# Expert stage on Trainium2: x2's sums in steps, rounding next to its ReLU, two products of h in the second product's banks, three banks for it, first copies by ScalarE

## What is computed

```python
def _moe2_ref(x, w_gate, w1, w2):          # x 3072x384, w1 8x384x1024, w2 8x1024x384
    logits = x @ w_gate
    logits = logits - logits.max()
    P = np.exp(logits)
    for _ in range(8):
        P /= P.sum(1, keepdims=True) + 1e-09
        P /= P.sum(0, keepdims=True) + 1e-09
        P *= N / E
    out = np.zeros((N, D), dtype=np.float32)
    for e in range(E):
        h = np.maximum(x @ w1[e], 0.0)
        ye = h @ w2[e]
        out += P[:, e:e + 1] * ye
    return out
```

## Time and profile before

| | us |
|---|---|
| runs of the kernel before | 2412.17, 2411.98, 2409.96 |
| median | 2411.98 |
| the profiled execution: time / span | 2413.01 / 2411.2 |
| TensorE matmuls busy in the span | 2256.0 |
| VectorE / ScalarE / GpSimd busy | 1743.3 / 979.0 / 503.9 |
| mean granted TensorE clock, share of full | 0.985 |

### The profile page before, as it was taken

The page is one execution under the profiler, slowest core; times in us unless marked ns, Lnnn a source line. Parts: engine busy times, 40 slices in busy tenths (PEclk is TensorE's granted clock), DMA queues, the critical chain, the costliest instruction groups (busy, mean ns, idle before and its releaser), DMA issues.

```text
span 2411.2 us, 38296 instructions
## 1 busy us (share of the span) xinstructions
PE 2256.0 (94%) x13723; PEld 2084.9 (86%) x13723; DVE 1743.3 (72%) x3098; ACT 979.0 (41%) x1669; POOL 503.9 (21%) x325
## 2 busy tenths in 40 slices
PE   2699999999998989999998999999998999999999
PEld 2689999999998878888887888888887888888888
DVE  6888888888864676666776676666667666766665
ACT  3455555555554333333333333333333333333332
POOL 0000000000000222232331233223232223332232
PEclk9799999999999999999999999999999999999999
DMA  3211111111112221111111121111101210111111
GB/s 105 82 42 51 49 48 48 48 47 48 47 35 93 65 80 53 53 52 39 40 52 53 53 105 53 53 52 52 50 28 52 79 51 29 53 52 53 52 53 27
DMA packets 70727, 131.35 MB, mean 54 GB/s; under 512 B 5512, under 2 KB 36488, under 8 KB 70536
## 3 DMA queue, kind: packets, MB, share of 16 engines
q1 hardware_dynamic: 70536, 129.14, 16.2%
HBM read 114.96 MB, written 14.16 MB: 54 GB/s over the span
## 4 chain that ended last, share of the span: by engine, by line
issue 41%; PE 29%; DVE 11%; POOL 11%; ACT 8%; POOLq 0%; DMA 0%; DVEq 0%; ACTq 0%; SPq 0%
POOL h_l L553 6%; PE bank L1402 5%; POOL w_l L548 5%; PE bank L1404 5%; PE bank L1403 5%; PE bank L1562 2%; PE bank L1564 2%; PE bank L1563 2%; PE bank L1383 2%; PE bank L1389 2%; PE bank L1388 2%; PE bank L1393 1%; ACT ubuf L637 1%; ACT ubuf L639 1%; ACT ubuf L635 1%
## 5 line engine op out<-in xcount | busy, mean ns | idle before, releaser
L1562 PE MATMUL bank<-w_h,h_h 128*128 128x384 f32 x1536 | 526.8, 343 | 38.5 <-DVE acc L1221 22.3
L1564 PE MATMUL bank<-w_h,h_l 128*128 128x384 f32 x1536 | 517.8, 337 | 0.0
L1563 PE MATMUL bank<-w_l,h_h 128*128 128x384 f32 x1536 | 517.5, 337 | 0.0
L553 POOL TENSOR_TENSOR h_l<-u_s,h_h 128x512 fp32r<-128x512 f32 x192 | 244.6, 1295 | 1046.9 <-ACT h_h L768 1046.9
L1402 PE MATMUL bank<-x_h,w_h 128*128 128x512 f32 x1056 | 414.7, 393 | 3.4 <-DVE h_l L1200 3.4
L1403 PE MATMUL bank<-x_l,w_h 128*128 128x512 f32 x1056 | 414.3, 392 | 0.0
L1404 PE MATMUL bank<-x_h,w_l 128*128 128x512 f32 x1056 | 413.2, 391 | 0.0
L1221 DVE SCALAR_TENSOR_TENSOR acc<-bank,prob,acc 128x384 f32<-128x384 f32 x352 | 215.9, 614 | 252.5 <-PE bank L1564 252.5
L1562 PEld LDWEIGHTS bank<-w_h,h_h 128*128 128x128 f32 x1536 | 291.1, 189 | 63.3 <-POOL h_l L553 29.3
L757 ACT ACTIVATE p_s<-bank 128x512 f32<-128x512 f32 x96 | 57.5, 599 | 603.9 <-PE bank L1404 603.9
L1563 PEld LDWEIGHTS bank<-w_l,h_h 128*128 128x128 f32 x1536 | 291.2, 190 | 2.0
(11 more groups left out here) (163 smaller groups left out, 4118.0 us busy)
## 6 DMA issues: line engine op xcount, KB each, us to landing
stage<-w_ SPq DMA_DIRECT2D x48, 768.0 KB, 6.5
w_raw<-w_ SPq DMA_DIRECT2D x96, 384.0 KB, 3.5
qb<-q_in_ SPq DMA_DIRECT2D x24, 192.0 KB
kb<-k_in_ SPq DMA_DIRECT2D x24, 192.0 KB
vb<-v_in_ SPq DMA_DIRECT2D x24, 192.0 KB
x_hi<-x2h_s SPq DMA_DIRECT2D x36, 128.0 KB, 1.8
x_lo<-x2l_s SPq DMA_DIRECT2D x36, 128.0 KB, 1.8
x_h<-x_hi SPq DMA_DIRECT2D x3, 1536.0 KB, 11.0
```

Source lines behind the costliest of these rows:

```text
L553: pool.tensor_tensor(tiles_of(h_l, name), group_sum(name), tiles_of(h_h, name).bitcast(F32), ALU.subtract).then_inc(hl_done, 1)
L1562: pe.matmul(dst, h_h[:, f, t_], w2h[:, fw], start=n == 0, stop=False)
L1563: pe.matmul(dst, h_h[:, f, t_], w2l[:, fw], start=False, stop=False)
L1564: mm = pe.matmul(dst, h_l[:, f, t_], w2h[:, fw], start=False, stop=n == 3)
```

## The change

Five edits, of which none changes a sum's terms. (1) `xt_sums` and `xt_lo` take a step: the eleven sums stand as 2, 2, 2, 2, 2 and 1 ahead of the additions k = 2 to 7 of groups 14 and 30, the five low parts one each ahead of the additions k = 0 to 4 of groups 15 and 31 (before: 1 and 4 tiles in two instructions). In stage B they stand at steps 4 and 5, and 6 and 7. (2) ScalarE rounds 22 right behind its ReLU, ahead of the ReLU of 12. (3) `h_bank` puts 11_0 and 21_0 in banks 6 and 7, and the second half in the banks of the first; the waits of `h_block` are written anew for that, with one for all additions of the group before, ahead of 11_0. (4) From group 2 on the second product uses banks 6, 7 and 2 by turns (`y_bank`), and tile k waits for the addition of tile k-3. (5) In group 0 ScalarE makes the copies into acc (L820 of the changed kernel), behind its rounding of w1 and w2, and in groups 0 and 1 GpSimd makes the low parts of the next w1, ahead of those of w2.

```diff
-                  "11_0": bank[0], "21_0": bank[1],
-                  "p1_1": bank[4], "p6_1": bank[5], "p5_1": bank[3], "p7_1": bank[0], "12_1": bank[1],
-                  "11_1": bank[4], "21_1": bank[5]}
+                  "11_0": bank[6], "21_0": bank[7],
+                  "p1_1": bank[0], "p6_1": bank[1], "p5_1": bank[3], "p7_1": bank[4], "12_1": bank[5],
+                  "11_1": bank[0], "21_1": bank[1]}
...
+        def in_sink(g):
+            return isinstance(g, int) and g < 2
+        def y_bank(g, k):
+            return yc[k % 2] if in_sink(g) else (bank[6], bank[7], bank[2])[k % 3]
...
# GpSimd, group
                 if nxt or j == 0:
+                    if in_sink(g):
+                        w1_lo(g + 1, 1 - j)
                     w2_lo(g + 1, 1 - j)
...
# ScalarE, group (the same for the second half)
                 relu(g, "22_0")
+                h_hi(g, "22_0")
                 relu(g, "12_0")
-                h_hi(g, "22_0")
                 h_hi(g, "12_0")
...
                     w2_hi(ex + j, g + 1, 1 - j)
+                if zero:
+                    for k, m in enumerate(M_ORDER):
+                        if k == 0:
+                            for n in range(KT):
+                                act.wait_ge(x2_stored[n], 32 * GROUPS)
+                        act.wait_ge(y2_full, k + 1)
+                        act.activation(acc[:, m], y_bank(0, k)[:, 0:DM], ACT.Copy).then_inc(acc_done, 1)
                 if x2_next:
                     xt_hi(x2_next)
...
# VectorE, group
-                    if x2_next and k == 4 * j:
-                        (xt_sums, xt_lo)[j](x2_next)
+                    if x2_next and j == 0 and k > 1:
+                        xt_sums(x2_next, k - 2)
+                    if x2_next and j and k < 5:
+                        xt_lo(x2_next, k)
...
-                    if (nxt or j == 0) and 1 < k < 5:
+                    if (nxt or j == 0) and 1 < k < 5 and not in_sink(g):
                         w1_lo(g + 1, 1 - j, (k - 2,))
-                    add_expert(g, j, k, ps, e)
+                    if not first:
+                        add_expert(g, j, k, ps, e)
...
# TensorE, h_block
-                if not zero:
-                    pe.wait_ge(sum_done, back + SUM["u3_1"])
                 product("p1_0", j, ps, ((W_11, X_11),))
-                if not zero:
-                    pe.wait_ge(sum_done, back + SUM["12_1"])
                 product("p6_0", j, ps, ((S_2, T_2),))
                 product("p5_0", j, ps, ((S_1, T_1),))
-                if not zero:
-                    pe.wait_ge(hl_dve, g * len(LOW_DVE) - 1)
                 product("p7_0", j, ps, ((S_3, T_3), (W_23, X_32)))
...
+                if not zero:
+                    pe.wait_ge(acc_done, g * PB)
+                product("11_0", j, ps, ((W_12, X_21), (W_13, X_31)))
+                product("21_0", j, ps, ((W_22, T_4), (W_23, D_3)))
                 pe.wait_ge(p1_kept, g * 2 + 1)
...
-                pe.wait_ge(hl_dve, g * len(LOW_DVE) + LOW_DVE["11_0"])
                 product("p7_1", j, ps, ((S_3, T_3), (W_23, X_32)))
...
# TensorE, y_block
-                    if k >= 2 or not zero:
-                        pe.wait_ge(acc_done, g * PB + k - 1)
+                    if k == 0:
+                        pe.wait_ge(hl_dve, g * len(LOW_DVE) + LOW_DVE["21_0"])
+                    behind = 2 if in_sink(g) else 3
+                    if k >= behind:
+                        pe.wait_ge(acc_done, g * PB + k - behind + 1)
```

More of the change, by code:

```diff
@@ L549, in w2_lo, with w1_lo @@
                                        ALU.subtract).then_inc(w2_low, 1)
+            def w1_lo(g, j):
+                raw_ = quad(j)
+                h, l, to = w1s[j]
+                for part, (w, r_) in enumerate(((slice(W_11, W_22), raw_[:, :, :, 0]),
+                                                (slice(W_22, S_1), raw_[:, 1:3, :, 1]),
+                                                (slice(S_1, NW), to[:, S_1:NW]))):
+                    pool.wait_ge(w1_high, g * 3 + part + 1)
+                    pool.tensor_tensor(l[:, w], r_, h[:, w].bitcast(F32), ALU.subtract).then_inc(w1_low, 1)
             def h_lo(g, name):
@@ L1107, in xt_lo @@
-            def xt_lo(ps):
+                if step < 2:
+                    dve.wait_ge(x2_in[ps % 2], 32 * (ps // 2 + 1))
+                    for a, b in ((T_1, X_11), (T_3, T_3), (T_2, X_22), (T_4, X_21))[2 * step:2 * step + 2]:
+                        dve.tensor_tensor(to[:, a], high[:, b], low[:, b], ALU.add).then_inc(xt_sum, 1)
+                elif step == 2:
+                    dve.tensor_tensor(to[:, D_3], high[:, X_31], high[:, X_32], ALU.subtract).then_inc(xt_sum, 1)
+                    dve.wait_ge(xt_sum, n + 4)
+                    dve.tensor_tensor(to[:, T_1], to[:, T_3], to[:, T_1], ALU.subtract).then_inc(xt_sum, 1)
+                elif step == 3:
+                    dve.tensor_tensor(to[:, T_3], to[:, T_2], to[:, T_3], ALU.subtract).then_inc(xt_sum, 1)
+                    dve.wait_ge(xt_sum, n + 6)
+                    dve.tensor_tensor(to[:, T_2], to[:, T_2], to[:, T_1], ALU.subtract).then_inc(xt_sum, 1)
+                elif step == 4:
+                    dve.wait_ge(xt_sum, n + 8)
+                    dve.tensor_tensor(to[:, D_3], to[:, D_3], low[:, X_31], ALU.add).then_inc(xt_sum, 1)
+                    dve.tensor_tensor(to[:, T_4], to[:, T_4], to[:, T_2], ALU.subtract).then_inc(xt_sum, 1)
+                else:
+                    dve.wait_ge(xt_sum, n + 9)
+                    dve.tensor_tensor(to[:, D_3], to[:, D_3], low[:, X_32], ALU.subtract).then_inc(xt_sum, 1)
@@ L1108, in xt_lo @@
+            def xt_lo(ps, step):
                 h, l, to = x2s[ps % 2]
-                for i, b in enumerate((slice(T_3, T_3 + 1), slice(T_1, NX))):
-                    dve.wait_ge(xt_high, 2 * ps + i + 1)
-                    dve.tensor_tensor(l[:, b], to[:, b], h[:, b].bitcast(F32), ALU.subtract).then_inc(xt_low, 1)
+                b = (T_3, T_1, T_2, T_4, D_3)[step]
+                dve.wait_ge(xt_high, 2 * ps + (2 if step else 1))
+                dve.tensor_tensor(l[:, b], to[:, b], h[:, b].bitcast(F32), ALU.subtract).then_inc(xt_low, 1)
@@ L1166, in _ @@
                     w1_lo(0, 0)
-                if m == 4:
-                    xt_sums(0)
-                if m == 6:
-                    xt_lo(0)
+                if m in (4, 5):
+                    for step in range(3):
+                        xt_sums(0, 3 * (m - 4) + step)
+                if m >= 6:
+                    for step in ((0, 1, 2), (3, 4))[m - 6]:
+                        xt_lo(0, step)
             g_lo(GROUPS * TILES - 1)
@@ L1204, in add_expert @@
                 m = M_ORDER[k]
-                y2, token = yc[k % 2][:, 0:DM], ps * PB + m
+                y2, token = y_bank(g, k)[:, 0:DM], ps * PB + m
                 dve.wait_ge(y2_full, g * PB + k + 1)
-                if e is None and j == 0 and ps == 0:
-                    for n in range(KT):
-                        dve.wait_ge(x2_stored[n], 32 * GROUPS)
-                    dve.tensor_copy(acc[:, m], y2).then_inc(acc_done, 1)
-                    return
                 if e is None and j == 0:
@@ L1491, in h_block @@
                 zero, one = (isinstance(g, int) and g == i for i in range(2))
-                here, back = g * len(SUM), (g - 1) * len(SUM)
+                here = g * len(SUM)
                 pe.wait_ge(w1_low, g * 3 + 3)
                 if first:
-                    pe.wait_ge(xt_low, 2 * (ps + 1))
-                if not zero:
-                    pe.wait_ge(sum_done, back + SUM["u3_1"])
+                    pe.wait_ge(xt_low, 5 * (ps + 1))
                 product("p1_0", j, ps, ((W_11, X_11),))
-                if not zero:
-                    pe.wait_ge(sum_done, back + SUM["12_1"])
                 product("p6_0", j, ps, ((S_2, T_2),))
                 product("p5_0", j, ps, ((S_1, T_1),))
-                if not zero:
-                    pe.wait_ge(hl_dve, g * len(LOW_DVE) - 1)
                 product("p7_0", j, ps, ((S_3, T_3), (W_23, X_32)))
@@ L1533, in h_block @@
                     pe.matmul(sk[:, 0:1], ones[0:1, :], gmax[0:1, 1:2], start=True, stop=True).then_inc(sink_pe, 1)
-                pe.wait_ge(hl_dve, g * len(LOW_DVE) + LOW_DVE["21_0"])
+                pe.wait_ge(sum_done, here + SUM["12_0"])
                 product("12_1", j, ps, ((S_4, X_22), (W_13, X_32)))
```

28 lines of the change are left out of this document (5 added, 23 removed).

## The result

The changed kernel takes 2384.02 us (median; 2383.05 to 2384.95), the kernel before beside it 2411.48: a ratio of 0.9882, with an interval of 0.987 to 0.9894. It is 27.5 us faster. The forecast was 2366, with 2384 as the upper end of the range: the direction held, the sum was 18 us too large, and the time lies on the very edge of the range. The profiled execution has a span of 2381.5 us against 2411.2.

A forecast was written before the change was run, and what follows sets the result against it. TensorE's matmuls, busy 94% of 2411.2 us, bound the kernel, so only its waits and lower-clock time could be won: 18.9 + 4 + 3 + 25.9 - 6 = 45.8 us, giving 2366 us, range 2350 to 2384.

The forecast's parts named there:

- Rounding sooner: Ordinary groups: rounding 22_1 ahead of 12_1's ReLU starts GpSimd 0.47 us sooner; 42 x 0.45 = 18.9 us won.
- Rival (c): Second half of groups: ScalarE's later 12_1 rounding becomes last, so 18.9 us shrinks to 5; 2380 us, chance 0.14.
- Three banks: Ordinary y blocks, third to sixth tile: 18 small waits for VectorE's additions go; 4 us won, between 3 and 4.5.
- H11 and H21: h blocks: banks 6 and 7 remove matmuls' waits for VectorE's low parts of 11 and 21; 3 us won (2 to 4).
- x2's sums in steps: Four y blocks at the two pass boundaries: 32.7 us loss less 3.4 kept per boundary; 25.9 us won (20 to 31).
- The first groups: Groups 0 and 1: ScalarE's late copies and VectorE standing behind GpSimd cost 6 us (+2 to -14).
- (d): Port lock costs more: -14 us in the first groups, 20 won at the boundaries; 2380 to 2385 us, chance 0.09.

The follow-up runs named there:

- the written-out ones: Changed kernel and kernel before, each with VectorE's three loops over the experts written out, other engines' loops kept: 2369.21 us and 2402.97 us.

## Why the prediction was right, and where it was 18 us too large

The direction was right, and most mechanisms. The sum of 45.8 us was 18.3 too large for the looped kernels, and 12.0 for the written-out ones (33.8). By its own steps:

- **Rounding sooner** (18.9): 19.0, or 17.6 where the term counted it. In the changed kernel the chain of the second half of a group stands as worked out, GpSimd 1.37 us behind the first ReLU's start and not 1.84 (both rows are of group 3):

```profile
932.63 0.63 ACT L779 ACTIVATE u_s<-u_s 128x512 f32<-128x512 f32 x1 [3.24 <-DVE u_s L1223]
933.29 0.63 ACT L786 ACTIVATE h_h<-u_s 128x512 fp32r<-128x512 f32 x1
...
934.00 2.54 POOL L569 TENSOR_TENSOR h_l<-u_s,h_h 128x512 fp32r<-128x512 f32 x2 [5.16 <-ACT h_h L786]
```

  Rival (c), that the margin of 0.1 us is not enough, did not come about.
- **Three banks** (4): right for ordinary groups, 4.6 us in the looped kernel. What the term left out is that it also absorbs the lateness that the steps leave, 6.9 us; and it did not see that the small waits come from the loops. Alone on written-out code it was not tried.
- **H11 and H21** (3): 0 to 2. Written out, the kernel before has 0.6 us of these waits and not 3.9.
- **x2's sums in steps** (25.9): this term failed as a term. The four boundary groups together did gain 25.6 us, and the y blocks came out at 17.95 and 18.79 where 18.3 and 18.5 were worked out. But that is the joint gain of several edits: the steps have 11 to 12 of it, the third bank 7, rounding sooner 2, the looped code in the kernel before 3. The prediction went from the whole loss straight to what should be left, and so hid that the banks' term was part of it. What should be left was worked out well: the four y blocks take 73.9 us together, where 73.6 was foretold, and the late rounding of x2 costs the second groups 2.1 to 2.4 us each, where 1.9 was. Between the written-out kernels the four groups gain 21.7 us.
- **The first groups** (-6): -6.7 in the trace of the looped kernels, -4.5 written out. The price of GpSimd's hold on VectorE, 2.2 us, was measured as 2.16, and the wait at the third tile, foretold as 6.3 and ended by ScalarE's copy, was 6.7. What was wrong is whom it blamed: ScalarE's place for the copies is worth nothing measurable. By the section of the Trainium skill that the prediction names ("SBUF — State Buffer", section "Who interferes with whom"), a `tensor_scalar` can enter modes that take the shared ports as well; the trace agrees, 1.67 for 0.18 us with a single input.
- **What had no term**: where VectorE's code stands, and what its jumps cost. This step failed most. In all groups but the first two and the four of the boundaries, the terms for rounding, banks and H promised 18.9 + 4 + 3 = 25.9 us, and the trace has 18.4 - 7.2 = 11.2: 14.7 are missing. VectorE's loops cost the changed kernel 14.8 us in these groups, but that is not the whole answer, since they cost the kernel before 7.5. Both written out, the same groups gain 18.5 us, little more than rounding sooner gives by itself. So 7.3 of the 14.7 are loops that cost more after the change, at the starts of their rounds, and 7.4 are terms that were too large: the terms for banks and H were read from waits that the loops of the kernel before cause. (The other 3.6 of the 18.3: 1.3 in the boundaries, the first groups and the start of the stage, and 2.3 in the two profiled executions: that of before took 1.5 more than its median, that of after 0.8 less.)

Rivals (c) and (d) named times near 2380, but for none of the reasons that the runs show.

What stays open is the rule by which the place decides. The body of VectorE's loop has 361 instructions. A packet of 8192 bytes seems to hold 128 of them: that is about how many VectorE passes from one packet to the next in the written-out kernel (119, 125, 128 and 128 at its end). Counted in its program, modulo 128 and from a zero that is arbitrary, the body begins at 84, 45 and 6 in the three passes of the kernel before, at 57, 21 and 113 after the change, at 87, 51 and 15 with 30 instructions more. The loss per round was small (0.5 to 1.3 us) at 84, 6, 57, 113, 87 and 51, nothing with no packet at all at 45, and 1.8 to 5.1 at 21 and 15 (up to 6.1 at 21 with two banks). At 21 the second stand comes 4 instructions into the body in both rounds, at 15 it comes 12 into it, again in both: 25 and 27, nearly the same place. This fits a page border there, where the loop's start has only few instructions in the page to which the jump leads, so that VectorE waits for two pages in turn. It is a conjecture from nine loops, and it does not say why nothing is fetched at 45; I had no run that sets the place freely.

## What to carry to other kernels

Judge a reordering of a looped kernel with and without the loop of the engine that is latest in its chain: here the same edits were worth 33.8 us written out and 27.5 looped, and thirty idle instructions moved two groups by 8 us together. Before small waits are priced, look whether they are there with the loops written out: some 7 us of them were the loops' own. When one stall is cut by several edits, price them together and then each on top of the others, since their single gains do not add up (11 or 12, and 7, of 25.6). Before GpSimd is given work to relieve VectorE, look at what VectorE runs in those microseconds: it stood 2.16 us behind two subtractions that would have taken it 1.55.

## What the runs showed of the hardware that was not expected

VectorE's jump back to the start of its loop made the group behind it from 0 to 5.1 us longer; with nothing changed but the place of the code, group 22 went from 4.6 us of loss to 0.8. A trace shows it as idle time marked "issue", or put on an engine that had long been done, next to packets of kind "instruction" (three around the start of group 22). Without such packets "issue" means something else: 2.51 us of it, twice, stayed in the kernel without jumps. A loss of VectorE of 5.6 us (2.61 + 2.98) reached TensorE as 4.6, part of it on the lower clock: the whole of group 22 has a mean granted clock of 0.95, where its neighbours have 1.00. And a TENSOR_SCALAR on 24 columns took 1.67 us next to a subtraction of GpSimd.
